# Token MLP of a three-part kernel: the order of the first token tile, and the PSUM banks of the transposes of x

## The reference

```python
# 1. clustered attention, for each of 2 x 8 heads: softmax(q k' / 8, only where the clusters agree) v
out = np.matmul(attn, v)
x = attn_out.transpose(0, 2, 1, 3).reshape(B, S, H * D)
# 2. token MLP, then channel MLP
xt = x.transpose(0, 2, 1)
h = np.maximum(xt @ w_tok1, 0.0) @ w_tok2        # w_tok1 768 x 256, w_tok2 256 x 768
u = x + h.transpose(0, 2, 1)
h2 = np.maximum(u @ w_ch1, 0.0) @ w_ch2          # w_ch1 512 x 1536, w_ch2 1536 x 512
x = u + h2
# 3. a rotation by x @ w_theta, two 768 x 768 token mixings, and a last 512 x 512 product
```

## Time and profile before

| | |
|---|---|
| times of the runs | 699.09, 699.20 and 701.43 us, median 699.2 us |
| profiled execution: its own time | 700.45 us |
| its span, from the first to the last instruction | 698.6 us |
| mean granted TensorE clock | 0.993 |
| TensorE matmuls busy | 679.3 us, 97% of the span |
| VectorE, ScalarE, GpSimd busy | 391.5, 338.5, 191.8 us |
| the seam and the token MLP | 277.9 to 323.4 us of the span |

### The profile page before, as it was taken

One profiled execution on the slowest core, in us unless ns is written; L12 is line 12 of the kernel. 1 busy time (PEld: TensorE's weight loads), 2 busy tenths in 40 slices (PEclk: granted clock), 3 DMA queues, 4 the chain that ended last, 5 costly groups with the idle time before them and its releaser, 6 DMA issues.

```text
span 698.6 us, 11568 instructions
## 1 busy us (share of the span) xinstructions
PE 679.3 (97%) x4188; PEld 643.6 (92%) x4188; DVE 391.5 (56%) x673; ACT 338.5 (48%) x641; POOL 191.8 (27%) x140
## 2 busy tenths in 40 slices
PE   7999999999999998999999999999999999999998
PEld 6888898989898987889999999999999999999998
DVE  6698888888897988445212202403268626671133
ACT  4687878787978788424401201301277425530010
POOL 5558253443535374402600000200223200060000
PEclk8999999999999999999999999999999999999999
DMA  6474644535353451100300000010231100000022
GB/s 218 87 177 122 170 100 103 135 68 135 68 135 68 100 149 46 32 14 20 125 9 0 1 1 0 0 45 1 59 122 50 57 1 1 0 1 1 1 90 91
DMA packets 16016, 45.44 MB, mean 65 GB/s; under 512 B 2544, under 2 KB 4592, under 8 KB 15984
## 3 DMA queue, kind: packets, MB, share of 16 engines
q1 hardware_dynamic: 15984, 45.00, 23.9%
HBM read 24.15 MB, written 3.15 MB: 39 GB/s over the span
## 4 chain that ended last, share of the span: by engine, by line
PE 87%; ACT 4%; DVE 4%; issue 3%; DMA 0%; ACTq 0%; DVEq 0%; SPq 0%
PE ps L439 19%; PE ps L441 19%; PE ps L440 19%; PE ps L477 7%; PE ps L485 5%; PE ps L469 4%; PE ps L486 4%; PE ps L470 4%; PE ps L450 3%; PE ps L461 1%; DVE pt_lo L1067 1%; ACT pt_hi L758 1%; ACT prob L783 1%; ACT kb L778 1%; PE ps L492 1%
## 5 line engine op out<-in xcount | busy, mean ns | idle before, releaser
L1039 DVE TENSOR_REDUCE neg_max<-ps 128x1 f32<-128x768 f32 x96 | 91.5, 954 | 27.4 <-PE ps L470 24.5
L1067 DVE TENSOR_TENSOR pt_lo<-ps,pt_hi 128x384 fp32r<-128x384 f32 x192 | 97.5, 549 | 11.2 <-ACT pt_hi L758 10.8
L758 ACT ACTIVATE pt_hi<-ps 128x384 fp32r<-128x384 f32 x192 | 84.4, 489 | 38.1 <-PE ps L477 36.6
L783 ACT ACTIVATE prob<-ps,neg_max 128x768 f32<-128x768 f32 x96 | 86.7, 904 | 13.1 <-DVE neg_max L1039 11.9
L867 ACT ACTIVATE g_s<-ps 128x384 fp32r<-128x384 f32 x48 | 23.6, 492 | 139.4 <-PE ps L441 139.4
L441 PE MATMUL ps<-u_s,ch_s 128*128 128x384 f32 (+1 forms) x256 | 85.5, 334 | 0.0
L439 PE MATMUL ps<-u_s,ch_s 128*128 128x384 f32 (+1 forms) x256 | 85.5, 334 | 0.0
L440 PE MATMUL ps<-u_s,ch_s 128*128 128x384 f32 (+1 forms) x256 | 85.5, 334 | 0.0
L477 PE MATMUL ps<-ident,prob 128*128 128x128 f32 x576 | 82.9, 278 | 1.4 <-DVE pt_lo L1067 1.3
L477 PEld LDWEIGHTS ps<-ident,prob 128*128 128x128 f32 x576 | 67.0, 143 | 10.6 <-DVE pt_lo L1067 2.7
L485 PE MATMUL ps<-pt_lo,v_s 128*128 128x384 f32 x192 | 70.2, 366 | 4.8 <-DVE o_sum L1046 4.8
(11 more groups left out here) (143 smaller groups left out, 1419.7 us busy)
## 6 DMA issues: line engine op xcount, KB each, us to landing
stage<-ch_dram SPq DMA_DIRECT2D x9, 768.0 KB, 4.3
qa<-pair_s SPq DMA_DIRECT2D x30, 192.0 KB, 2.8
ka<-pair_s SPq DMA_DIRECT2D x30, 192.0 KB, 3.8
raw<-q_dram SPq DMA_DIRECT2D x8, 384.0 KB, 4.2
raw<-k_dram SPq DMA_DIRECT2D x8, 384.0 KB, 4.6
raw_v<-v_dram SPq DMA_DIRECT2D x8, 384.0 KB, 4.3
out_dram<-act_u SPq DMA_DIRECT2D x16, 192.0 KB, 1.9
qb<-pair_s SPq DMA_DIRECT2D x15, 192.0 KB, 3.4
```

The costliest lines, as they stand in the source:

```text
L758: return act.activation(o, i, ACT.Copy)
L783: act.activation(prob[:, slot, :].rearrange("p (c k) -> p c k", c=2), ps[:, 2 * slot:2 * slot + 2, 0:HS], ACT.Exp, bias=neg_max[:, s:s + 1 ...
L1039: dve.tensor_reduce(neg_max[:, s:s + 1], ps[:, 2 * slot2:2 * slot2 + 2, 0:HS], AX.XY, ALU.max, negate=True).then_inc(s_max, 1)
L1067: dve.tensor_tensor(pt_lo[at], ps[:, 4 + u, 0:HS].rearrange("p (k q) -> p k q", k=HT), pt_hi[at], ALU.subtract).then_inc(s_pt_lo, 1)
```

## The change

Two edits are made. The computation stays the same, and no instruction is added or removed; some move, and the semaphores that some wait for change.

First, token tile 0 of batch 0 is taken out of its row of six. Its split is put into the last step (`s` = 11) of the last attention pair on ScalarE and VectorE, and its six matmuls (`token_in(0, 0)`) stand ahead of the `weighted_v` of half-head 31. `o_transpose` of half-head 31 comes behind tile 3, not behind tile 2. Second, the transposes of x rotate over six banks (`XT_BANK`), so that only groups 6 and 7 wait for a copy, and the waits that protected banks 4 to 7 move from the second token product to the transposes. The second product's first four groups wait for the copies out of those banks.

```diff
+        XT_BANK = (2, 3, 4, 5, 6, 7)
...
+            def x_transposes(b):
                 for i in range(2 * DT):
                     half, d = i // DT, i % DT
                     n = 2 * DT * b + i
-                    if n >= 2:
-                        pe.wait_ge(s_xt, n - 1)
+                    if i >= len(XT_BANK):
+                        pe.wait_ge(s_xt, n - len(XT_BANK) + 1)
+                    elif b:
+                        pe.wait_ge(s_u, 2 * DT * b)
+                        pe.wait_ge(s_xt, 2 * DT * b)
+                    elif i == 2:
+                        pe.wait_ge(s_pt_lo, 2 * NG)
+                    elif i == 4:
+                        pe.wait_ge(s_x_bank, 4 * NP)
+                    elif i == 5:
+                        pe.wait_ge(s_koh, 2 * NP)
                     for t in range(HT):
-                        mm = pe.transpose(ps[:, 2 + i % 2, t * P:(t + 1) * P],
+                        mm = pe.transpose(ps[:, XT_BANK[i % len(XT_BANK)], t * P:(t + 1) * P],
...
+            def token_out(b):
                 arrived(pe, W_TOK2)
                 pe.wait_ge(s_h, JT * b + JT)
...
-                    if n < 2:
-                        pe.wait_ge(s_pt_lo, 2 * NG)
-                    elif n == 2:
-                        pe.wait_ge(s_x_bank, 4 * NP - 1)
-                    elif n == 3:
-                        pe.wait_ge(s_koh, 2 * NP)
+                    if i < 4:
+                        pe.wait_ge(s_xt, 2 * DT * b + i + 3)
                     else:
                         pe.wait_ge(s_u, n - 3)
...
+            token_in(0, 0)
+            pe.wait_ge(s_pt_lo, 12 * 2 * NP)
+            pe.wait_ge(s_x_bank, 4 * NP - 1)
+            weighted_v(1, 1, 0)
+            weighted_v(1, 1, 1)
+            for t in range(1, NT):
+                token_in(0, t)
+                if t == 3:
+                    pe.wait_ge(s_ot, 4 * NP)
+                    o_transpose()
+            x_transposes(0)
+            token_out(0)
+            for t in range(NT):
+                token_in(1, t)
+            x_transposes(1)
+            token_out(1)
...
             def pair(p, first=False, last=False):
                 for s in range(12):
...
+                    if last and s == 11:
+                        act.wait_ge(s_score, NG)
+                        act.wait_ge(s_x, 4 * 4)
+                        x_hi(0, 0)
...
+                    if last and s == 11:
+                        x_lo(0, 0)
```

More of the change, by code:

```diff
@@ L586, in _, with token_in @@
             pair(NP - 1, last=True)
-            pe.wait_ge(s_pt_lo, 12 * 2 * NP)
-            pe.wait_ge(s_x_bank, 4 * NP - 1)
[L589 to L610, removed]
+            def token_in(b, t):
+                pe.wait_ge(s_xs, NT * b + t + 1)
+                if t == 0:
+                    arrived(pe, W_TOK1)
+                    pe.wait_ge(s_exp, NG)
+                    if b:
+                        pe.wait_ge(s_h, JT * b)
+                xs = [x_s[:, i, :].rearrange("p (h t c) -> p h t c", h=4, t=NT)[:, :, t, :] for i in range(2)]
+                for j in range(JT):
+                    ws = [tok1_s[:, i, t, j * P:(j + 1) * P] for i in range(2)]
+                    mm = product(ps[:, j, :].rearrange("p (h c) -> p h c", h=4), ws[0], ws[1], xs[0], xs[1],
+                                 t == 0, t == NT - 1)
+                    if t == NT - 1:
+                        mm.then_inc(s_h_pe, 1)
+            def x_transposes(b):
                 for i in range(2 * DT):
@@ L788, in o_out, with x_hi @@
                 copy(o_t[:], ps[:, 6, 0:HS]).then_inc(s_ot, 1)
+            def x_hi(b, t):
+                view = "p (h t c) -> p h t c"
+                copy(x_s[:, 0, :].rearrange(view, h=4, t=NT)[:, :, t, :],
+                     x_tok[:, 4 * b * NT:4 * (b + 1) * NT, :].rearrange("p (h t) c -> p h t c", h=4)[:, :, t, :]
+                     ).then_inc(s_xs_hi, 1)
             def pair(p, first=False, last=False):
@@ L834, in _ @@
                     act.wait_ge(s_h_pe, JT * b)
[L835 to L838, removed]
+                    act.wait_ge(s_x, 4 * 4 * (b + 1))
+                for t in range(0 if b else 1, NT):
                     if b == 0 and t == 3:
                         o_out(4 * NP - 1)
[L841 to L844, removed]
+                    x_hi(b, t)
                 if b:
@@ L853, in _ @@
                     act.wait_ge(s_xt_pe, 2 * DT * b + i + 1)
-                    copy(x_t[:, i // DT, i % DT, :], ps[:, 2 + i % 2, 0:HS]).then_inc(s_xt, 1)
+                    copy(x_t[:, i // DT, i % DT, :], ps[:, XT_BANK[i % len(XT_BANK)], 0:HS]).then_inc(s_xt, 1)
             def u_hi(c, slot):
@@ L1052, in half_out, with x_lo @@
                 dve.reciprocal(rden[:, half, :], rden[:, half, :]).then_inc(s_rden, 1)
+            def x_lo(b, t):
+                dve.wait_ge(s_xs_hi, NT * b + t + 1)
+                view = "p (h t c) -> p h t c"
+                hi, lo = (x_s[:, i, :].rearrange(view, h=4, t=NT)[:, :, t, :] for i in range(2))
+                xv = x_tok[:, 4 * b * NT:4 * (b + 1) * NT, :].rearrange("p (h t) c -> p h t c", h=4)[:, :, t, :]
+                dve.tensor_tensor(lo, xv, hi, ALU.subtract).then_inc(s_xs, 1)
             def pair(p, first=False, last=False):
@@ L1087, in _ @@
             pair(NP - 1, last=True)
[L1090 to L1095, removed]
             def u_lo(c, slot):
@@ L1101, in u_lo @@
                                   parts[:, bass.ds(slot * 2 * CH, CH)], ALU.subtract).then_inc(s_us, 1)
-            for t in range(NT):
+            for t in range(1, NT):
                 x_lo(0, t)
```

## The result

The changed kernel takes 695.12 us in the median of six runs (694.54 to 695.97), the kernel before 699.5 us (698.89 to 701.43); the ratio is 0.9939, with a 95% interval of 0.9929 to 0.9949. By the ratio that is 4.3 us or 0.61% faster (the two medians are 4.4 us apart), where 4.5 us and 694.7 us were forecast. Of the 0.4 us between 694.7 and 695.12, 0.3 is that the forecast started from a median of 699.2 us and not 699.5.

What follows compares the result with a forecast made beforehand. TensorE's instruction stream (busy 679.3 of 698.6 us) was taken as the bound. Savings of 1.39 + 3.08 = 4.47 us, about 4.5 off the 699.2 us median, gave 694.7 us, range 693.6 to 697.3.

Steps and rivals of the forecast that it cites:

- Term 1: At the seam, tile 0's six matmuls fall into TensorE's gap ahead of the last weighted sum: -1.39 us.
- The insertion at 0: In the last attention step, tile 0's copy and subtraction fit idle times of ScalarE and VectorE: cost 0, at most 1.30 us.
- the first rival: At the seam, tile 0 comes late, its 1.30 us insertion delaying o_sum: gain 3.2 us, 696.0 us; chance 8%.
- the collision: Tile 0's VectorE subtraction took 0.996 us beside GpSimd's x_tok write, otherwise 0.68; after the change tile 1 meets it.
- Term 2: Over the transposes of x, six banks cut 4.18 us to 2.64 per batch: -1.54 us each, -3.08 us.
- the other end of the range: Transposes of x at the attention's pitch of 0.095 us: 24 take 2.3 us, the six-bank term is -3.8 us.
- The three waits: Groups 6 and 7 and the second product find their copies (and h_s) done before TensorE gets there.
- the copies' pace: Over the transposes of x, ScalarE's 0.385 us copies set the pace: 3.1 us a batch, gain 3.6 us; chance 8%.
- Nothing behind takes it back: From the channel MLP on, no gap swallows the shift; the rival, another wait leaving under 2 us, had 5%.
- The clock: Rival: over the dense transposes and after, granted clock falls to 0.50, 702.7 us or more; chance 3%.
- The sum: Whole kernel: 1.39 + 3.08 = 4.47 us less than the profiled execution.

Runs made afterwards that it cites:

- The three-fold subtraction: The full change with VectorE doing token tile 0's subtraction three times in the last attention step; 696.34 us, one run.
- seam too: Against the kernel before: the change, plus o_sum ahead of the argmax in attention step 5 and between the two pt_lo in the last step; 694.00 us, ratio 0.9918.
- 96 transposes: The full change with each group of three transposes of x in batch 0 done four times; 703.58 us, one run.

## Why the prediction was right

**Term 1, tile 0 in the gap: -1.39 predicted, -1.36 measured** between the fixed points of the run with that edit alone. The matmuls lie where the arithmetic put them, with 0.2 us of idle time behind rather than 0.25.

**The insertion at 0.** Measured 0: `o_t` and the weighted sum kept their distances. The three-fold subtraction shows that this was a matter of fit and not of indifference; the first rival's mechanism exists, with a threshold that this change stays 0.2 us below (I had put it at 0.1, because I counted on ScalarE, but not on VectorE, that consecutive instructions overlap by some 0.1 us). The margin was thin, and that it held was partly luck. The subtraction took 0.68 us, away from GpSimd, as assumed. But I had read the collision one instruction too early: before the change the subtraction that started at 279.40 (tile 0) took 0.66 us, and the one behind it (tile 1) took the 0.996. So in the changed kernel it is tile 2 that meets it, with 0.994 us, and tile 1 takes 0.66. In the kernel "seam too" GpSimd's write started first and took 0.51 us; the first subtraction beside it took 0.77 and the second 0.68:

```profile
277.78 0.51 POOL L386 TENSOR_TENSOR x_tok<-o_sum,rden 128x192 f32<-128x192 f32 x1 [5.17 <-DVE rden L1074]
...
278.06 1.37 DVE L1081 TENSOR_TENSOR x_s<-x_tok,x_s 128x512 fp32r<-128x512 f32 x2
```

In the changed kernel, where the first subtraction is under way when GpSimd's write starts, it is 0.86 us for the write and 1.57 for the two:

```profile
279.26 1.57 DVE L1080 TENSOR_TENSOR x_s<-x_tok,x_s 128x512 fp32r<-128x512 f32 x2
279.42 0.86 POOL L386 TENSOR_TENSOR x_tok<-o_sum,rden 128x192 f32<-128x192 f32 x1 [5.63 <-DVE rden L1073]
```

So whichever starts first keeps its length, and the next one of the other engine is longer. That agrees with the rule of the Trainium skill named in the prediction ("SBUF — State Buffer", Who interferes with whom).

**Term 2, six banks: -3.08 predicted, -3.23 measured.** The size was off by 0.15 us: 24 transposes take 2.54 us and not 2.64. The pitch was right, (2.78 - 0.27) / 23 = 0.109 us, but the matmul behind the last transpose starts 0.03 us after it (291.10 and 291.13), so 24 of them take 23 pitches and not 24. The pitch of 0.095 that I took from the earlier trace rows for the other end of the range is the same thing: five pitches of 0.11 and 0.02. The three waits were all met, and the model of the round (1.12 us) and of the copies' pace (0.385 us) gave the times of three and four banks within 0.03 us.

**Nothing behind takes it back.** The channel MLP started at 318.73 with no idle time in front, 4.73 us earlier; of that 0.15 us was there before the seam.

**The clock.** Granted 1.00 over the whole seam, and over 96 transposes too. In the prediction a rule of the Trainium skill spoke for a fall ("TensorE: Matmul & The Clock Gate", PE-mode transpose); the trace doesn't bear it out here: with matmuls before and behind, a row of 10.4 us of fp32 transposes left the granted clock at 1.00.

**The sum.** 4.47 predicted, 4.58 between the fixed points, 4.3 us from the ratio (3.6 to 5.0).

## What to carry to other kernels

A wait on the bounding engine is worth just the work that can be put in front of it. Look for such work in the next stage, and pay for its preparation in idle times of the same step on the other engines; a second serving there costs nearly its full length. For a ring of buffers compute two numbers, the round of one buffer divided by their count and the pace of the engine that empties them; the larger one is the pace of a long row. If the writer is faster than the emptying engine and the row is short, further buffers still help, since the writer runs ahead in them: of the 0.53 us between three and six banks the fourth brought all but 0.14. Swapping two instructions on a loaded engine moved three quarters of a wait in the attention (0.12 of 0.47 us were kept) and kept its 0.29 us at the seam, where no row maximum stood behind it; taking one out of the crowded step into an idle time removed the rest.

## What was not expected of the hardware

ScalarE's copies look longer when they queue back to back: the `x_t` copies have a median of 528 ns in the changed kernel and 490 ns before, but eight of them take 3.17 us, a pitch of (3.17 - 0.53) / 7 = 0.377 us, against 0.38 us within the pairs of the earlier trace rows. A longer record was no slower engine here, so the cost of a copy in a row is read from the starts; what makes it longer stays open. Half a microsecond of difference between two profiled executions came from stretches with identical code, and the mean granted clock of the first 30 us was 0.83 in some profiles and 0.89 or 1.00 in others.
